# Throwaway products on TensorE in a fused mLSTM, routed-expert and soft-expert kernel, and late weight loads in column halves

## Chip, cores and metric

One Trainium2 chip, one core. The metric is device time in microseconds of one execution, as the median of several runs.

## The reference

Three stages, all in float32. Stage one is a gated linear-attention recurrence over 768 tokens, for 4 batches and 8 heads of 40 channels; stage two sends each of the 3072 tokens to one of 8 experts; stage three is a soft mixture over 32 slots.

```python
for t in range(S):                                    # stage one
    m_new = np.maximum(f_gate[:, :, t] + m, i_gate[:, :, t])
    C = f_stab * C + i_stab * outer(v_t, k_t);  n = f_stab * n + i_stab * k_t
    y_t = sigmoid(o_t) * (C @ q_t) / np.maximum(np.abs(n @ q_t), 1.0)
# stage two, x is (3072, 320)
expert_idx = np.argmax(x @ w_gate, axis=1)
out[mask] = gate_w[mask, None] * (np.maximum(x[mask] @ w1[e], 0.0) @ w2[e])
# stage three
logits = x @ phi                                      # (3072, 32)
slot_input = softmax(logits, axis=0).T @ x            # (32, 320)
slot_out[e] = np.maximum(slot_input[e] @ v1[e], 0.0) @ v2[e]   # 4 slots per expert
y = softmax(logits, axis=1) @ slot_out
```

w1 and v1 are 8 matrices of 320 x 1024, w2 and v2 of 1024 x 320.

## The kernel before

Each engine has its own hand-written program; semaphores join them. SyncE issues nearly all DMAs.

**Stage one** goes in 24 steps (6 chunks of 128 tokens by 4 batches, chunks outside). VectorE first works the gates through scans, from which it builds the operands of the first exponent product. For a step TensorE runs `exponents` (L1164, two products of 512 columns, whose results ScalarE puts through Exp and GpSimd masks), `scores` (L1176), `outputs` (L1187 for the carried state, from the second chunk on, and L1192), `new_state` (L1203) and `x_transpose` (L1209). VectorE weighs the scores with the decays (L883) before the outputs can run. After the first scores `gate_columns` transposes gate rows (L1245, L1248). Once in four steps come `router` (L1229) and `logit_transpose` (L1237).

**Routing** follows on one path through TensorE and VectorE: one-hot choice (`r_hot`), the rank products L1281 and L1282 (`r_rank`), positions and row masks on VectorE (L982), 24 slot products L1288 (`r_slots`), slot numbers to GpSimd, which gathers the rows of the tokens by indirect DMA; beside that the gate products L1374 (`slot_gates`, 10 of them before the first tile, 14 after its first layer).

**The expert loop** takes 31 tiles of 128 slots. Weights and activations are split in a high and a low fp32r part, and each product is made of three (L1315 to L1319 for layer 1, L1332 to L1334 for layer 2). It is the same before and after.

**The tail** is stage three: the column maximum (L1428, L1430), the slot inputs (L1437 over 31 tiles, four column tiles side by side, with the sums L1441 in between), a fold (L1447), then for two groups q of four experts `soft1` (L1461), `soft_transpose` (L1471), `soft2` (L1482), with `transpose_combine` (L1489) between the groups, a spreading product (L1502) and 24 final products L1511, which VectorE and ScalarE scale and SyncE stores.

The soft experts' weights go to places that become free: experts 6 and 7 into the places of experts 0 and 1, once `soft1(0)` has read them (`soft_h` at 2). `soft1(q)` waits for the whole w1 of its four experts and then makes the columns in two halves g of 512, each into a bank of its own. Before a stage's wait the program does nothing: `pe.wait_ge` stands there and TensorE is idle. Bank 6 is free until the first carried state, and again between the routing's products and the gates; bank 4 holds the ranks and, later, layer 2; bank 2 is free between the slot sums and the transposes.

The semaphore `consts` is raised by GpSimd as soon as the identity, the ones and `half` are made (L461 to L468).

Of the kernel before, what the change touches and what calls it, by code (L numbers as in the profile page):

```python
# [29 lines left out]
P = 128  # L30
# [16 lines left out]
def build(nc, i_gate, f_gate, qk_rows, kvo_rows, w_gate, phi, w1_main, w1_rest, w2, v1_main, v1_rest, v2, out):  # L47
    B, H, S = i_gate.shape
    DM, E = w_gate.shape
# [22 lines left out]
    with ExitStack() as ctx:  # L72
# [216 lines left out]
        soft_in = [[sem(f"soft_w1_in{n}"), sem(f"soft_w2a_in{n}"), sem(f"soft_w2b_in{n}")] for n in range(E)]  # L289
# [62 lines left out]
        def _(sp):  # L352
# [39 lines left out]
            def load_soft_w1(e):  # L392

                raw, there = soft_place(e), soft_in[e][0]
                sp.dma_start(raw[:, 0:2 * F], v1_main[e]).then_inc(there, 16)
                sp.dma_start(raw[0:KD[2][1], 2 * F:W1N], v1_rest[e]).then_inc(there, 16)

            def load_soft_w2(e, halves=(0, 1)):
                for x in halves:
                    a, z = x * W2N // 2, (x + 1) * W2N // 2  # L400
                    sp.dma_start(soft_place(e)[:, W1N + a:W1N + z], v2[e][:, a:z]).then_inc(soft_in[e][1 + x], 16)
# [40 lines left out]
            load_soft_w1(6)  # L442
            load_soft_w1(7)
# [705 lines left out]
        def _(pe):  # L1149
            mm = nc.tensor.matmul  # L1150
            tr = nc.tensor.transpose
            def exponents(i):

                c, b = ORDER[i]
                if c == 0:
                    pe.wait_ge(exp_first, 1)
                    pe.wait_ge(exp_const, 2)
                else:
                    pe.wait_ge(exp_next, c)
                    pe.wait_ge(exp_const, 4)  # L1160
                if i > 0:
                    pe.wait_ge(dec_raw, i)
                for a in range(2):
                    last = mm(bank[a][:, :], exp_cols[c % 2][:, b, :],  # L1164
                              exp_rows[c % 2][:, a * NP:(a + 1) * NP, :].rearrange("p n t -> p (n t)"), start=True, stop=True)
                last.then_inc(e_done, 1)
# [85 lines left out]
            pe.wait_ge(consts, 1)  # L1252
            exponents(0)
# [24 lines left out]

            pe.wait_ge(r_hot, 1)
# [3 lines left out]

            pe.wait_ge(r_row, 1)
# [93 lines left out]

            pe.wait_ge(r_gates_split, 1)
# [3 lines left out]
            gathered(0, 0, 0)  # L1383
            layer1(0, 0, at0)
# [41 lines left out]

            pe.wait_ge(cmax_in, 1)
            tr(bank[0][0:SLOTS, 0:P], cmx[:, :], ident[:, :]).then_inc(cmax_tr, 1)  # L1428
            pe.wait_ge(cmax_dg, 1)
            mm(bank[1][:, 0:SLOTS], ones[0:SLOTS, :], cdg[:, :], start=True, stop=True).then_inc(cmax_bc, 1)  # L1430
            pe.wait_ge(e_exp, 1)
            pe.wait_ge(y_kept, TILES)
            for j in range(TILES):
                if j == E_PARTS[1][0]:
                    pe.wait_ge(e_exp, 2)
                i = j % GRP * SLOTS
                last = mm(bank[3][i:i + SLOTS, 0:DM], et[:, j, :], ys3[:, j, :], start=(j < GRP), stop=(j >= TILES - GRP))  # L1437
                if j == TILES // 2:
                    pe.wait_ge(e_sum, 1)
                    for i in range(GRP):  # L1440
                        summed = mm(bank[2][i * SLOTS:(i + 1) * SLOTS, 0:1], esum[:, :], ones[:, 0:1], start=True, stop=True)  # L1441
                    summed.then_inc(sl_sum, 1)
# [8 lines left out]
            def soft1(q):  # L1451
                for e in range(GRP * q, GRP * (q + 1)):
                    pe.wait_ge(soft_in[e][0], 32)
                for g in range(2):
                    if q > 0:
                        pe.wait_ge(soft_relu[g], q)
                    for kk in range(3):
                        n = KD[kk][1]
                        for i in range(GRP):
                            e = GRP * q + i  # L1460
                            last = mm(bank[g][i * SLOTS:i * SLOTS + PER, :], s_T[0:n, kk, PER * e:PER * (e + 1)],  # L1461
                                      soft_place(e)[0:n, kk * F + g * 512:kk * F + (g + 1) * 512], start=(kk == 0), stop=(kk == 2))
# [11 lines left out]
            def soft2(q):  # L1474
                pe.wait_ge(hs_ready, 2 * q + 2)
                for kk in range(NF):
                    if kk % (NF // 2) == 0:
                        for e in range(GRP * q, GRP * (q + 1)):
                            pe.wait_ge(soft_in[e][1 + kk // (NF // 2)], 16)
# [15 lines left out]
            transpose_combine()  # L1495
            soft1(1)
# [48 lines left out]

# [26 lines left out]
```

## Time and profile before

| | us |
|---|---|
| median of 3 runs | 611.08 |
| lowest and highest run | 603.78, 613.95 |
| the profiled execution's own time | 603.99 |
| its span in the profile | 602.2 |
| TensorE busy | 523.0 (87%) |
| VectorE, ScalarE, GpSimd busy | 325.1, 194.1, 328.0 |
| mean granted TensorE clock | 0.921 |

The stages lie in the span thus: gates until 19.4, chunk steps until 203, routing until 228.6, expert loop until 537, tail until the end. A granted clock of 1.00 is 2.4 GHz, one of 0.50 is 1.2 GHz. The clock column has no level of its own for the time before the first recorded change, at 63.1 us, and shows 1.00 there; the lengths of the products tell it. An fp32 product appears as two records of TensorE; `x16` counts records.

### The profile page before, as it was taken

How to read it: one execution, taken by the hardware profiler on the slowest of the kernel's cores; microseconds unless marked ns; L12 is line 12 of the kernel's file. 1: busy time of each engine (PE TensorE's matmuls, PEld its weight loads, DVE VectorE, ACT ScalarE, POOL GpSimd, SP SyncE). 2: the span in 40 equal slices, each digit the busy share in tenths (PEclk: the TensorE clock that was granted, in tenths of full speed). 3: DMA queues.
4: the chain of work that ended last, by engine and by line, in shares of the span. 5: the costliest groups of instructions: out<-in, count | busy, mean ns of one | idle time of the engine just before them, and what ended most of it. 6: DMA issues, size and time to landing. Idle time of an engine off the chain costs nothing.

```text
span 602.2 us, 11312 instructions
## 1 busy us (share of the span) xinstructions
PE 523.0 (87%) x3819; PEld 443.8 (74%) x3820; DVE 325.1 (54%) x547; ACT 194.1 (32%) x424; POOL 328.0 (54%) x301
## 2 busy tenths in 40 slices
PE   0599999989999258999999999999999999979483
PEld 0389888878898146989898898989888989862222
DVE  7445677876744573634747757574554333342113
ACT  2233554646630221232333323232323232220003
POOL 2465768778644315755997868685297442102000
PEclk9999999999755557999999999999999999998887
DMA  6026789888720004348160606050230650039927
GB/s 207 0 67 218 222 264 272 266 260 266 232 86 22 11 18 114 89 111 223 68 213 16 208 22 202 22 202 22 90 117 20 213 182 16 2 114 359 340 92 262
DMA packets 28447, 86.22 MB, mean 143 GB/s; under 512 B 4464, under 2 KB 14816, under 8 KB 25344
## 3 DMA queue, kind: packets, MB, share of 16 engines
q1 hardware_dynamic: 21616, 75.07, 38.5%
q0 software_dynamic: 2480, 5.59, 3.7%
q10 hardware_dynamic: 4320, 5.15, 2.5%
q8 instruction: 20, 0.33, 0.2%
q14 instruction: 11, 0.09, 0.0%
HBM read 72.67 MB, written 8.37 MB: 135 GB/s over the span
## 4 chain that ended last, share of the span: by engine, by line
PE 73%; DVE 13%; issue 5%; DMA 4%; POOL 2%; ACT 1%; SPq 0%; DVEq 0%; ACTq 0%; POOLq 0%
PE bank L1192 8%; PE bank L1332 7%; PE bank L1334 6%; PE bank L1333 6%; PE bank L1315 5%; PE bank L1209 5%; PE bank L1317 4%; PE bank L1316 4%; PE bank L1176 4%; PE bank L1343 4%; PE bank L1187 3%; PE bank L1357 3%; DVE gates L1040 2%; PE bank L1319 2%; PE bank L1461 2%
## 5 line engine op out<-in xcount | busy, mean ns | idle before, releaser
L1332 PE MATMUL bank<-W_high,h_high 128*128 x248 | 79.1, 319 | 1.7 <-DVE h_low L1065 1.6
L626 POOL TENSOR_TENSOR W_high<-W,ones 128x3072 fp32r<-128x3072 f32 (+1 forms) x12 | 58.6, 4885 | 37.8 <-PE bank L1334 37.7
L1334 PE MATMUL bank<-W_low,h_high 128*128 x248 | 76.4, 308 | 0.0
L1333 PE MATMUL bank<-W_high,h_low 128*128 x248 | 76.4, 308 | 0.0
L592 POOL TENSOR_TENSOR W_low<-W,W_high 128x3072 fp32r<-128x3072 f32 (+1 forms) x12 | 74.9, 6238 | 0.9
L776 ACT ACTIVATE h_high<-bank 128x512 fp32r<-128x512 f32 x62 | 33.7, 595 | 123.7 <-PE bank L1343 119.5
L874 DVE RECIPROCAL hb<-hb 128x320 f32<-128x320 f32 x24 | 51.7, 2153 | 27.9 <-POOL hb L530 27.9
L635 POOL DMA_INDIRECT combine_slots<-gates,back_i x31 | 29.8, 960 | 60.3 <-ACT gates L764 37.3
L1192 PE MATMUL bank<-ys 128*128 128x41 f32 x384 | 59.4, 325 | 0.0
L1192 PEld LDWEIGHTS bank<-ys 128*128 128x128 f32 x384 | 57.9, 238 | 0.9 <-issue 0.9
L1315 PE MATMUL bank<-W_high,x_high 128*128 x124 | 52.8, 426 | 4.9 <-DVE x_high L1048 2.5
L1021 DVE TENSOR_TENSOR yc<-bank,slot_gate 128x320 f32<-128x320 f32 x31 | 15.2, 492 | 75.4 <-PE bank L1334 75.4
L1053 DVE TENSOR_SCALAR hb<-bank 128x512 f32<-128x512 f32 x31 | 21.3, 688 | 55.4 <-PE bank L1319 55.4
L1040 DVE TENSOR_TENSOR gates<-gates,rmx (+1 forms) x31 | 50.5, 1631 | 0.0
L1317 PE MATMUL bank<-W_low,x_high 128*128 x124 | 49.3, 398 | 0.0
L1316 PE MATMUL bank<-W_high,x_low 128*128 x124 | 49.3, 397 | 0.0
L1332 PEld LDWEIGHTS bank<-W_high,h_high 128*128 128x128 f32 x248 | 46.6, 188 | 2.4 <-issue 2.4
L1333 PEld LDWEIGHTS bank<-W_high,h_low 128*128 128x128 f32 x248 | 46.6, 188 | 0.0
L1334 PEld LDWEIGHTS bank<-W_low,h_high 128*128 128x128 f32 x248 | 46.5, 188 | 0.0
L609 POOL DMA_INDIRECT ys<-x_tokens,slot_i x29 | 32.2, 1112 | 25.7 <-DMA ys<-x_tokens,slot_i 22.8
L1065 DVE TENSOR_TENSOR h_low<-bank,h_high 128x512 fp32r<-128x512 f32 x62 | 39.7, 681 | 5.5 <-ACT h_high L776 5.5
L1176 PEld LDWEIGHTS bank<-ys 48*128 48x128 f32 x384 | 30.5, 238 | 13.7 <-issue 11.4
(245 smaller groups left out, 1090.6 us busy)
## 6 DMA issues: line engine op xcount, KB each, us to landing
W<-in_moe_w_main_dram SPq DMA_DIRECT2D x13, 1024.0 KB, 6.0
ys<-in_kvo_rows_dram SPq DMA_DIRECT2D x24, 484.0 KB, 5.5
ys<-in_qk_columns_dram SPq DMA_DIRECT2D x24, 448.0 KB, 4.2
W<-in_moe_w_rows_dram SPq DMA_DIRECT2D x8, 1280.0 KB, 9.2
W<-in_moe_w_rows_dram SPq DMA_DIRECT2D x10, 640.0 KB, 8.8
W<-in_moe_w_rest_dram SPq DMA_DIRECT2D x21, 256.0 KB, 6.7
xs<-ys ACTq DMA_DIRECT2D x29, 160.0 KB, 2.1
x_tokens<-xs SPq DMA_DIRECT2D x24, 160.0 KB, 4.9
```

Source lines behind the costliest of these rows:

```text
L592: g.tensor_tensor(W_low[:, w], W[:, w], W_high[:, columns(e % 2, part_)].bitcast(F32), ALU.subtract).then_inc(w_split[part_], 1)
L626: g.tensor_tensor(W_high[:, columns(e % 2, part_)], w, ones[:, 0:1].broadcast_to(list(w.shape)), ALU.mult).then_inc(high_ready, 1)
L874: v_.reciprocal(eo[i % 3], eo[i % 3]).then_inc(recip_ready, 1)
L1040: v_.tensor_tensor(a(cexp), a(lg2), m.unsqueeze(2).broadcast_to([P, 1, SLOTS]), ALU.subtract).then_inc(c_in, 1)
L1176: last = mm(bank[3 + a][:, n * P:(n + 1) * P], qkT[i % 3][r, 1, n, :], qkT[i % 3][r, 0, n, :], start=True, stop=True)
L1192: last = mm(bank[5][:, h * DA:(h + 1) * DA], pr[i % 2][h % 2][:, h // 2, :], vt[i % 3][:, h, :], start=True, stop=True)
L1315: mm(dst, x_high[n][:, kk, :], high, start=(kk == 0), stop=False)
L1316: mm(dst, x_low[n][:, kk, :], high, start=False, stop=False)
L1317: mm(dst, x_high[n][:, kk, :], w1_at(W_low, slot, kk, half_, P), start=False, stop=False)
L1332: mm(dst, h_high[:, kk, :], high, start=(kk == 0), stop=False)
L1333: mm(dst, h_low[:, kk, :], high, start=False, stop=False)
L1334: last = mm(dst, h_high[:, kk, :], w2_at(W_low, slot, kk), start=False, stop=(kk == NF - 1))
```

## The change

A helper is added to TensorE's program. It multiplies the identity by the identity, repeated four times to 512 columns, into a bank whose content nobody reads:

```diff
+            def keep_warm(n, free):
+                for _ in range(n):
+                    mm(free[:, :], ident[:, :], ident[:, :].unsqueeze(1).broadcast_to([P, 4, P]), start=True, stop=True)
...
             pe.wait_ge(consts, 1)
+            keep_warm(28, bank[6])
             exponents(0)
...
+            keep_warm(5, bank[6])
             pe.wait_ge(r_hot, 1)
...
+            keep_warm(14, bank[6])
             pe.wait_ge(r_row, 1)
...
+            keep_warm(8, bank[6])
             pe.wait_ge(r_gates_split, 1)
             slot_gates(0, 10)
             fetch(0)
             at0 = places(expert[0])
             gathered(0, 0, 0)
+            keep_warm(3, bank[4])
             layer1(0, 0, at0)
...
+            keep_warm(1, bank[2])
             pe.wait_ge(cmax_in, 1)
...
+            keep_warm(1, bank[2])
             pe.wait_ge(e_exp, 1)
...
                 if j == E_PARTS[1][0]:
+                    keep_warm(2, bank[2])
                     pe.wait_ge(e_exp, 2)
...
             transpose_combine()
+            keep_warm(10, bank[2])
             soft1(1)
```

These are 72 products. Where they stand on TensorE, at the start of its program (`bank<-ident` is the throwaway; L1164 before is L1170 now), before:

```order
L1148 UNCONDITIONAL_BRANCH
L1164 MATMUL bank<-exp_rows_53,exp_cols_55 128x512 x4
L1176 MATMUL bank<-ys 128x128 x8
L1245 MATMUL bank<-ident,gates 128x32 x12
L1248 MATMUL bank<-gates,half 128x96 x2
```

and now:

```order
L1149 UNCONDITIONAL_BRANCH
L1156 MATMUL bank<-ident 128x512 x28
L1170 MATMUL bank<-exp_rows_53,exp_cols_55 128x512 x4
L1182 MATMUL bank<-ys 128x128 x8
L1251 MATMUL bank<-ident,gates 128x32 x12
L1254 MATMUL bank<-gates,half 128x96 x2
```

All 28 stand ahead of the first exponent products; nothing else moved. The routing on TensorE, from the last logit transpose to the first layer-1 product, before:

```order
L1237 MATMUL bank<-ident,sin_ 128x128
L1281 MATMUL bank<-oh_bf,before_bf 128x192
L1282 MATMUL bank<-oh_bf,ones_bf 128x192
L1288 MATMUL bank<-token_hot,rowhot 128x64 x24
L1374 MATMUL bank<-gate_parts,rowhot 128x64 x10
L1365 TENSOR_LOAD eot_i
L1209 MATMUL bank<-ident,xs 128x128 x3
```

and now:

```order
L1243 MATMUL bank<-ident,sin_ 128x128
L1156 MATMUL bank<-ident 128x512 x5
L1289 MATMUL bank<-oh_bf,before_bf 128x192
L1290 MATMUL bank<-oh_bf,ones_bf 128x192
L1156 MATMUL bank<-ident 128x512 x14
L1297 MATMUL bank<-token_hot,rowhot 128x64 x24
L1156 MATMUL bank<-ident 128x512 x8
L1383 MATMUL bank<-gate_parts,rowhot 128x64 x10
L1374 TENSOR_LOAD eot_i
L1215 MATMUL bank<-ident,xs 128x128 x3
L1156 MATMUL bank<-ident 128x512 x3
```

Four groups of throwaways stand in the four waits. The other part of the change is the soft experts' w1. On the host its main part is laid out so that the first 512 columns of both row blocks come before the last 512. Each w1 is loaded by four DMAs instead of two, halves apart, and for experts 6 and 7 the first halves of both go first. For experts 4 to 7 each half has a semaphore of its own, and `soft1` waits for a half before the product g that reads it:

```diff
-            def load_soft_w1(e):
-
-                raw, there = soft_place(e), soft_in[e][0]
-                sp.dma_start(raw[:, 0:2 * F], v1_main[e]).then_inc(there, 16)
-                sp.dma_start(raw[0:KD[2][1], 2 * F:W1N], v1_rest[e]).then_inc(there, 16)
+            def load_soft_w1(e, halves=(0, 1)):
+                for x in halves:
+                    a, there = x * W1N // 2, soft_in[e][2 + x * (e // GRP)]
+                    sp.dma_start(soft_place(e)[:, a:a + F], v1_main[e][:, x * F:(x + 1) * F]).then_inc(there, 16)
+                    sp.dma_start(soft_place(e)[0:KD[2][1], a + F:a + W1N // 2], v1_rest[e][:, x * F // 2:(x + 1) * F // 2]).then_inc(there, 16)
...
             sp.wait_ge(soft_h, 2)
-            load_soft_w1(6)
-            load_soft_w1(7)
+            for x in range(2):
+                load_soft_w1(6, (x,))
+                load_soft_w1(7, (x,))
...
             def soft1(q):
-                for e in range(GRP * q, GRP * (q + 1)):
-                    pe.wait_ge(soft_in[e][0], 32)
                 for g in range(2):
+                    for e in range(GRP * q, GRP * (q + 1)):
+                        pe.wait_ge(soft_in[e][2 + q * g], 32 if q else 64)
```

## Rows read from the trace of the kernel before

**Rows 1.** Windows cut where the granted clock changes: busy us of each engine, PEclk, DMA share, GB/s

```profile
29.60:63.10 33.50, 33.47 (x218) 29.37 (x220) 17.77 (x24) 12.98 (x29) 20.49 (x41) 1.00 0.45 143
63.10:158.70 95.60, 88.87 (x1047) 78.73 (x1047) 71.74 (x107) 51.01 (x118) 72.00 (x113) 1.00 0.85 263
158.70:203.30 44.60, 38.81 (x236) 33.58 (x235) 20.44 (x27) 11.82 (x25) 24.33 (x27) 0.50 0.20 66
203.30:233.80 30.50, 14.28 (x51) 12.17 (x52) 18.75 (x49) 8.29 (x8) 7.51 (x7) 0.50 0.14 38
...
541.00:547.80 6.80, 5.78 (x54) 2.37 (x56) 2.24 (x4) 1.21 (x3) 4.35 (x8) 0.50 1.01 368
...
568.30:575.10 6.80, 3.60 (x20) 0.52 (x24) 0.00 (x0) 0.00 (x0) 0.00 (x0) 0.50 1.00 363
```

**Rows 2.** Timeline of GpSimd, first 3 us: start, length, what

```profile
2.46 0.14 POOL L468 MEMSET half<- 32x64 f32 x1
```

**Rows 3.** Timeline of TensorE, 18 to 62 us

```profile
19.36 1.19 PE L1164 MATMUL bank<-exp_rows,exp_cols 128*128 128x512 f32 x2 [19.36 <-DVE exp_cols L859]
...
29.63 2.08 PE L1176 MATMUL bank<-ys 48*128 48x128 f32 x16 [1.08 <-DVE ys L883]
31.64 3.63 PE L1192 MATMUL bank<-ys 128*128 128x41 f32 x16
```

**Rows 4.** The chain that ended last: start, length, what

```profile
20.59 1.09 ACT arena L656 x2
...
28.20 1.30 DVE ys L883 x2
...
64.55 1.75 PE bank L1192 x16
...
67.84 1.09 PE bank L1176 x16
...
161.39 2.01 PE bank L1176 x16
...
170.20 2.01 PE bank L1176 x16
```

**Rows 5.** Timeline of TensorE, chunk boundaries, 80 to 160 us

```profile
106.76 0.30 PE L1237 MATMUL bank<-ident,sin_ 128*128 128x128 f32 x1 [1.05 <-issue]
...
155.73 0.30 PE L1237 MATMUL bank<-ident,sin_ 128*128 128x128 f32 x1 [1.04 <-issue]
```

**Rows 6.** Timeline of TensorE, products of the tail, 551 to 587 us

```profile
551.38 0.60 PE L1461 MATMUL bank<-W,s_T 128*4 128x512 f32 x2 [0.41 <-DVE s_T L1123]
...
551.82 0.59 PE L1461 MATMUL bank<-arena,s_T 128*4 128x512 f32 x1
...
585.86 0.81 PE L1502 MATMUL bank<-gates,spread 128*128 128x320 f32 x2 [0.62 <-DVE gates L1139]
```

**Rows 7.** Timeline of TensorE, the routing

```profile
206.59 0.34 PE L1281 MATMUL bank<-oh_bf,before_bf 128*128 128x192 bf16 x1 [3.38 <-DVE oh_bf L948]
...
214.83 5.30 PE L1288 MATMUL bank<-token_hot,rowhot 128*128 128x64 f32 x24 [7.75 <-DVE rowhot L982]
222.52 2.34 PE L1374 MATMUL bank<-gate_parts,rowhot 128*128 128x64 f32 x10 [2.39 <-DVE gate_parts L1007]
225.99 0.90 PE L1209 MATMUL bank<-ident,xs 128*128 128x128 f32 x3 [1.12 <-DMA xs<-x_tokens,slot_i]
228.57 0.79 PE L1315 MATMUL bank<-W_high,x_high 128*128 x1 [1.68 <-DVE x_high L1048]
```

**Rows 8.** Timeline of TensorE, start of the tail

```profile
538.23 0.28 PE L1428 MATMUL bank<-ident,cmx 128*32 128x128 f32 x1 [0.51 <-DVE cmx L1097]
...
540.34 0.73 PE L1437 MATMUL bank<-ys,gates 128*32 128x320 f32 x4 [0.83 <-ACT gates L798]
542.09 3.95 PE L1437 MATMUL bank<-ys,gates 128*32 128x320 f32 x26 [1.02 <-ACT gates L798]
```

**Rows 9.** Timeline of TensorE, second w1 product of the tail

```profile
571.50 1.01 PE L1461 MATMUL bank<-arena,s_T 128*4 128x512 f32 x1 [7.27 <-DMA W<-in_moe_w_rest_dram]
```

More of the change, by code:

```diff
@@ L288, in build @@
         weights_in = sem("weights_in")
-        soft_in = [[sem(f"soft_w1_in{n}"), sem(f"soft_w2a_in{n}"), sem(f"soft_w2b_in{n}")] for n in range(E)]
+        soft_in = [[sem(f"soft_{part_}_in{n}") for part_ in ("w2a", "w2b", "w1a", "w1b")[:3 + n // 4]] for n in range(E)]
         dve_chain = sem("dve_chain")
@@ L400, in load_soft_w2 @@
                     a, z = x * W2N // 2, (x + 1) * W2N // 2
-                    sp.dma_start(soft_place(e)[:, W1N + a:W1N + z], v2[e][:, a:z]).then_inc(soft_in[e][1 + x], 16)
+                    sp.dma_start(soft_place(e)[:, W1N + a:W1N + z], v2[e][:, a:z]).then_inc(soft_in[e][x], 16)
             def load_soft(e):
@@ L1461, in soft1 @@
                             last = mm(bank[g][i * SLOTS:i * SLOTS + PER, :], s_T[0:n, kk, PER * e:PER * (e + 1)],
-                                      soft_place(e)[0:n, kk * F + g * 512:kk * F + (g + 1) * 512], start=(kk == 0), stop=(kk == 2))
+                                      soft_place(e)[0:n, g * W1N // 2 + kk * 512:g * W1N // 2 + (kk + 1) * 512], start=(kk == 0), stop=(kk == 2))
                     last.then_inc(soft_h, 1)
@@ L1478, in soft2 @@
                         for e in range(GRP * q, GRP * (q + 1)):
-                            pe.wait_ge(soft_in[e][1 + kk // (NF // 2)], 16)
+                            pe.wait_ge(soft_in[e][kk // (NF // 2)], 16)
                     for i in range(GRP):
@@ L1543, in _token_rows, with _by_column_halves @@
     return np.ascontiguousarray(np.concatenate([a.reshape(a.shape[0], P, -1) for a in parts], axis=2))
+def _by_column_halves(rows, parts):
+    split = rows.reshape(rows.shape[0], rows.shape[1], parts, 2, -1).transpose(0, 1, 3, 2, 4)
+    return np.ascontiguousarray(split.reshape(rows.shape))
 def kernel(**inputs):
@@ L1560 @@
         a = _np.asarray(inputs[first])
-        laid.append((first + "_main", _partition_rows(a[:, :2 * P])))
+        main = _partition_rows(a[:, :2 * P])
+        laid.append((first + "_main", _by_column_halves(main, 2) if first == "moe2_w1" else main))
         laid.append((first + "_rest", _np.ascontiguousarray(a[:, 2 * P:])))
```

## The prediction

> **What bounds the kernel now.** I read the page's 40 slices first, then a table of windows cut where the granted clock changes, then TensorE's timeline at each place where the change adds work. TensorE is 87% busy and the chain that ended last runs over it, so its speed decides. That speed is not constant. The windows [rows 1] show the clock at 1.00 from 63.1 to 158.7 us, 0.50 until 233.8, 1.00 through the expert loop, and two short stretches of 0.50 in the tail. Before 63.1 the column says 1.00 too, but there the records contradict it: the same sixteen products of L1192 take 3.63 us at 31.6 and 1.75 us at 64.6 [rows 3, 4]. So TensorE runs at 1.2 GHz until 63.1 and at 2.4 GHz after it. A chunk step takes 8.8 us at the lower level (two starts of L1176, 161.4 and 170.2) and at the higher 49.0 us for the eight steps between the logit transposes at 106.76 and 155.73, 6.1 each [rows 4, 5]. In the low stretch 29.6 to 63.1 TensorE is busy 33.47 of 33.50 us [rows 1]: there it is the bound, and a faster clock pays at once.
>
> **The sum's base.** The profiled execution took 603.99 us (span 602.2, 1.8 around it). The median shown is 611.08, 7.1 more, and the three runs lie 10.2 apart. Four steps at 8.8 instead of 6.1 are 10.8 us, so one chunk more or less at the low clock explains the spread. 2% of the median, about what a measurement of this kernel can tell from no change, is 12.2 us: faster means below 598.9, slower above 623.3.
>
> **What one throwaway costs.** No row shows it. The nearest is the one untiled fp32 product of 320 columns, L1502: two records that take 0.82 us together [rows 6]; the shorter of them lasts 0.43, so they start 0.39 apart, which is 0.62 for 512 columns if none of it is start-up. In L1461, with 512 columns and four small tiles side by side, the next pass over the same tile starts 0.44 us after the first (551.38 and 551.82) [rows 6]. I take 0.43 us per record and two records per product: 0.85 us at 2.4 GHz, 1.7 us at 1.2. The bounds are 0.43 (if one record did) and 1.24 (two records 0.62 apart). The identity is fp32, as L1502's operands are, so 0.85 is nearest.
>
> **Front, 28 of them.** They start when the fourth small memset is done at 2.6 us [rows 2] and stand ahead of exponents(0), which now starts at 19.36, released by VectorE. The first stretch of dense work after a low clock shows when it rises: from 228.57 to 233.8 is 5.2 us, from 571.5 to 575.1 is 3.6 us [rows 1, 7, 9]. I take 4.5 us, 2.6 products; the other 25.4 take 21.7 us. TensorE is free at 28.9 us, that is +9.5 us. (At 2.4 GHz throughout 26.6; at 1.24 each about 37.) Behind it the startup runs faster. Now 19.36 to 29.63 is 10.3 us: product, ScalarE's exponential, product, scores, gate columns, two copies and a weighing on VectorE [rows 3, 4]. With TensorE's pieces halved it is 0.6 + 1.1 + 0.6 + 1.1 + 1.2 + 0.2 + 0.8 + 1.3 = 6.9, so -3.4. Then five steps lie between the scores of step 1 at 29.63 and those of step 6 at 67.84: 38.2 us [rows 3, 4]. At the high clock a step costs at least 3.8 (half of 38.2 / 5) and at most the 6.1 of a later chunk, which has L1187 besides. I take 5.2: 26.0 us, -12.2. Front: 9.5 - 3.4 - 12.2 = -6.1 us, bounds -14 and 0.
>
> The cover of this term is the clock itself. From 4.8 us after the 28 until 6.9 us after them TensorE waits for VectorE, an idle of 2.1 us where it was 1.08, because the wait is VectorE's and does not shrink. The clock has gone through idles of 1.05 us at 105.7 unharmed and fell at 158.7 after one of 1.04 [rows 5]. The Trainium skill ("TensorE: Matmul & The Clock Gate", Part 4) says that transposes do not count as busy for the clock. Were that so here, the 12 gate-column transposes would lengthen the gap from the scores on, and the front would end at +6.2 instead of -6.1; no row separates transposes from the rest.
>
> **Chunk loop.** No instruction changes. I leave the fall at the end of the fifth chunk where it is: 0, with 0 to -14 if it does not fall (rival C).
>
> **Routing, 5 + 14 + 8 + 3.** TensorE's waits here are 3.38, 7.75, 2.39 + 1.12 and 1.68 us [rows 7]. The 5 start at 203.2 at the low clock: 4.5 us for 2.6 of them and 2.4 x 0.85 for the rest, 6.5 us, done at 209.7 against 206.6: +3.1, and the rank product and all of VectorE's chain behind it (7.95 us to the first rowhot) are late by that. The 14 take 11.9 us from 210.0, done at 221.9, while VectorE has its quarter ready at 217.9. The 24 slot products take 5.30 us now; at the high clock 2.7: 224.6 against 220.1, +4.5. The 8 take 6.8, the ten gate products 1.2: 232.6. The gathered rows come 5.9 us after the slots (220.1 to 226.0), at 230.5, so they are hidden. Three transposes 0.5 and the 3 throwaways 2.6: layer 1 starts at 235.7, +7.1 against 228.57. Its first ten or so products now take 5.2 us until the clock rises and will take 2.6. Net +4.5 us (bounds: -3 if everything fits in the waits, +7 if the clock is low again). The expert loop follows at 1.00 either way: shifted, not changed.
>
> **Tail, 1 + 1 + 2 + 10 and the halves.** The waits are 0.51, 0.83 and 1.02 us [rows 8]; against 0.85, 0.85 and 1.7 this delays by 0.3 + 0 + 0.7. In return the clock stays up where it is 0.50 from 541.0 to 547.8 [rows 1], and the L1437 groups (8 groups of four tiles, about 7.3 us with the sums between) take some 4.7: -2.6. Net about -1.6 before soft1(0). soft1(1) now waits 7.27 us, until 571.5, for the last rest load of w1 [rows 9]. The 10 take 8.5 us from 562.6, until 571.1; the first column halves of experts 6 and 7 have come by then, since the queues are full (1.02 of 16 engines) and half of the 2.5 MB is left. The second halves are there at about 571.3, as the whole was, and are wanted only 2.6 us later. soft1(1) takes 5.2 instead of 7.4 us and ends at 576.2 instead of 579.0: -2.8 us for the whole tail (the 1.6 is inside it). Bounds 0, if smaller packets slow the loads, and -5, if g = 0 could start early. SyncE issues 16 DMAs more, some 0.5 us each, while its queues hold work: nothing. What ends the kernel stays the output's transfer.
>
> **Sum.** 603.99 - 6.1 + 0 + 4.5 - 2.8 = 599.6 us for an execution whose chunk loop goes as the profiled one did. The median of before sits 7.1 higher for a rise that came late or a fall that came early; the 28 remove the first kind only. I add a third, 2.4: forecast 602.0, own range 593 to 609.
>
> **Rivals.**
> B, the clock falls in the startup gap. For: 2.1 us idle, twice today's, with little work ahead of it; the fall at 158.7 needed only 1.04 us and a thin stretch of L1192 behind it. Against: the same idle at 105.7 did nothing. The 28 then bought nothing: scores 1 at 35.8 instead of 29.63, +6.2, and the cold steps as now: 602 + 12.3 = 614. If the rise that came at 63 then comes a chunk later, 10.8 more: 625. It decides from the first fall before 40 us on. This is the one that ends slower than before.
> C, the clock does not fall at 158.7, since the phase of every idle has moved. Four steps at 6.1 instead of 8.8 and a quicker router, some 12.5 us, and the 5 throwaways enter at the high clock, 2.2 less: 602 - 15 = 587. For it: the boundary idles of the other chunks passed. Against it: nothing in the change touches this stretch.
> D, the throwaways are short, so they don't do what they say. At the lower bound, one record each, the 28 end near 13 to 15 us, the idle until 19.36 is over 4 us, and the clock fell in the idle after 564.2 after 4.1 us [rows 1, 9]. Nothing is gained in front, the routing's fit in the waits and cost nothing; tail -2.8, layer 1 -1.3: 611.1 - 4.1 = 607. The skill's same page (section on the back-to-back issue gap) gives N/2.4 + 2.5 ns, 0.216 us for 512 columns, which would put the 28 at under 10 us and the result at the same 607; the records of L1502 speak against it, and another page, "FP8 and Floating Point Precision", counts four passes for true fp32.
>
> **Chances.** Forecast 0.37; B 0.30, of it 0.11 beyond 623; C 0.18; D 0.07; the rest, mixtures such as a fall at the first chunk boundary (near 606 to 616), 0.08. Faster by over 2%: C, and a third of the forecast's own range, 0.30. Slower by over 2%: 0.12. Within: 0.58. The range leaves out the far ends of B and C: 587 to 621.
>
> **What would show it.** Right: L1164's first start near 29, L1192 at 1.75 us per sixteen from its first step on, scores 6 near 61, rank product 3 us behind the router, layer 1 some 7 us after today's distance from the router, soft1(1) done at the high clock. Wrong: throwaways that end the 28 before 20 us (D); L1192 at 3.6 us per sixteen in the first steps (B); windows at 1.00 up to the router (C). If the routing's waits still stand in the list of waits, my throwaway is too long by half.

## The result, and the profile after

| | before | after |
|---|---|---|
| median, us | 609.41 | 629.38 |
| lowest and highest of 4 runs, us | 603.78, 613.95 | 626.24, 639.45 |
| after / before | | 1.034, 95% interval 1.022 to 1.046 |

The change makes the kernel slower, by 20 us between the medians. The forecast was 602.0 us within 587 to 621. The profiled execution of after is the longest of its four, 639.45 us; the other three took 626 to 631. So its stages are read one by one below, and its chunk loop is not typical. The ratios with an interval, here and below, are taken from the fast runs alone, so they are not the quotients of the medians beside them, which are of all runs.

The page of after first. TensorE is busy for 76.8 us more than before, 68.5 of them the throwaways' own (144 records, 72 products), and the chain that ended last runs over those for 9% of the span.

```profile
span 637.6 us, 11620 instructions
...
PE 599.8 (94%) x3963; PEld 485.7 (76%) x3964; DVE 331.7 (52%) x547; ACT 195.1 (31%) x424; POOL 327.7 (51%) x301
...
PEclk9965569855559869999999999999999999999998
...
PE 82%; DVE 7%; issue 4%; DMA 2%; POOL 2%; ACT 1%; SPq 1%; DVEq 0%; POOLq 0%; ACTq 0%
...
L1156 PE MATMUL bank<-ident 128*128 128x512 f32 x144 | 68.5, 631 | 3.7 <-POOLq L470 2.7
```

Then the windows of after, cut where the granted clock changes, which answer to [rows 1] (columns: window, length, then busy us and number of records of TensorE, its weight loads, VectorE, ScalarE, GpSimd; clock; DMA share; GB/s). The column to look at is the clock: it rises at 8.0, while the 28 throwaways run, falls at 35.3, six microseconds after them, and stands at 0.50 until 89.9. Before, the low stretch ended at 63.1. It is low again from 124.0 to 192.3, with TensorE busy for 68.30 of 68.30 us. From 265.4 on it stays up until 632.6, through nearly the whole tail, where before it fell three times.

```profile
8.00:35.30 27.30, 25.91 (x89) 12.53 (x87) 12.09 (x15) 6.04 (x10) 8.06 (x16) 1.00 0.20 48
35.30:89.90 54.60, 53.16 (x338) 47.00 (x340) 28.01 (x40) 19.08 (x42) 32.83 (x59) 0.50 0.44 137
89.90:124.00 34.10, 32.14 (x387) 28.50 (x384) 25.09 (x38) 17.11 (x42) 23.81 (x38) 1.00 0.83 271
124.00:192.30 68.30, 68.30 (x457) 60.18 (x456) 34.40 (x50) 24.37 (x54) 34.87 (x55) 0.50 0.51 161
192.30:232.50 40.20, 32.23 (x321) 27.93 (x322) 24.66 (x34) 16.29 (x34) 26.82 (x32) 0.88 0.38 129
232.50:265.40 32.90, 31.88 (x100) 16.24 (x100) 18.74 (x49) 7.75 (x7) 6.56 (x6) 0.94 0.09 24
265.40:575.00 309.60, 302.69 (x1875) 271.69 (x1874) 168.75 (x283) 93.96 (x214) 188.91 (x78) 1.00 0.33 105
575.00:632.60 57.60, 48.17 (x402) 19.39 (x400) 14.94 (x34) 9.18 (x22) 4.36 (x8) 1.00 0.83 271
```

By stages, each from its first product to that of the next, in us of the profiled executions:

| stage | before | after | difference | forecast |
|---|---|---|---|---|
| start to scores of step 1 | 29.6 | 36.7 | +7.1 | +6.1 |
| scores of step 1 to last logit transpose | 173.1 | 195.5 | +22.4 | -12.2 |
| last logit transpose to layer 1 (routing) | 25.8 | 33.2 | +7.3 | +7.1 |
| layer 1 to column maximum (expert loop) | 309.7 | 309.7 | 0.0 | -2.6 |
| column maximum to end (tail) | 64.0 | 62.6 | -1.4 | -2.8 |
| span | 602.2 | 637.6 | +35.4 | |

(The routing's three parts are, before and after, 3.9 and 6.7 to the rank product, 8.2 and 11.8 to the slot products, 13.7 and 14.7 to layer 1. The table's rows add up to the span within rounding.)

### The profile page after: what moved, and what is told of

Its sections match the earlier page's. It is cut to its first block, busy times and chain, and to the rows that moved or that the text cites. A ratio compares the mean times of both kernels' runs of the same rounds, so it can differ in the third digit from the quotient of the medians.

```text
span 637.6 us, 11620 instructions
## 1 busy us (share of the span) xinstructions
PE 599.8 (94%) x3963; PEld 485.7 (76%) x3964; DVE 331.7 (52%) x547; ACT 195.1 (31%) x424; POOL 327.7 (51%) x301
## 4 chain that ended last, share of the span: by engine, by line
PE 82%; DVE 7%; issue 4%; DMA 2%; POOL 2%; ACT 1%; SPq 1%; DVEq 0%; POOLq 0%; ACTq 0%
PE bank L1156 9%; PE bank L1198 8%; PE bank L1341 6%; PE bank L1343 6%; PE bank L1342 6%; PE bank L1182 5%; PE bank L1324 5%; PE bank L1215 5%; PE bank L1326 4%; PE bank L1325 4%; PE bank L1193 4%; PE bank L1352 3%; PE bank L1366 3%; DMA W<-in_moe_w_rest_dram 2%; DVE gates L1041 2%
## 5 line engine op out<-in xcount | busy, mean ns | idle before, releaser
L1156 PE MATMUL bank<-ident 128*128 128x512 f32 x144 | 68.5, 631 | 3.7 <-POOLq L470 2.7
L1198 PE MATMUL bank<-ys 128*128 128x41 f32 x384 | 66.1, 347 | 0.0
L1198 PEld LDWEIGHTS bank<-ys 128*128 128x128 f32 x384 | 64.8, 263 | 0.9 <-issue 0.9
L1156 PEld LDWEIGHTS bank<-ident 128*128 128x128 f32 x144 | 28.5, 203 | 37.2 <-issue 34.8
L1041 DVE TENSOR_TENSOR gates<-gates,rmx (+1 forms) x31 | 56.6, 1830 | 0.0
L1182 PEld LDWEIGHTS bank<-ys 48*128 48x128 f32 x384 | 35.1, 270 | 15.2 <-issue 14.5
```

The lines of the kernel that those rows point to most:

```text
L1041: v_.tensor_tensor(a(cexp), a(lg2), m.unsqueeze(2).broadcast_to([P, 1, SLOTS]), ALU.subtract).then_inc(c_in, 1)
L1156: mm(free[:, :], ident[:, :], ident[:, :].unsqueeze(1).broadcast_to([P, 4, P]), start=True, stop=True)
L1182: last = mm(bank[3 + a][:, n * P:(n + 1) * P], qkT[i % 3][r, 1, n, :], qkT[i % 3][r, 0, n, :], start=True, stop=True)
L1198: last = mm(bank[5][:, h * DA:(h + 1) * DA], pr[i % 2][h % 2][:, h // 2, :], vt[i % 3][:, h, :], start=True, stop=True)
```

## The experiments

Sixteen kernels. Each is the kernel before with the helper and the edits named (e9 is the kernel after, e5 has no helper); e1 to e4 also mask the expert number that TensorE's loop reads (`pe.snap(e & 7)`), e5 to e16 instead hold the tile-to-expert table as 16-bit numbers. Neither changes a product or a load. e5 is the second edit alone, the control; the mask has no control of its own. Kernels of one group ran on one chip, with the kernel before beside them. The text of each expectation is as it was written before the run.

### One part at a time

e1 has the front's 28 alone, e2 the routing's four calls alone, e3 the tail's four and the column halves (as in the change's diff, whose other lines for the tail are left out):

```diff
# e1
             pe.wait_ge(consts, 1)
+            keep_warm(28, bank[6])
             exponents(0)
# e2
+            keep_warm(5, bank[6])
             pe.wait_ge(r_hot, 1)
...
+            keep_warm(14, bank[6])
             pe.wait_ge(r_row, 1)
...
+            keep_warm(8, bank[6])
             pe.wait_ge(r_gates_split, 1)
...
+            keep_warm(3, bank[4])
             layer1(0, 0, at0)
# e3
             transpose_combine()
+            keep_warm(10, bank[2])
             soft1(1)
```

> Only the 28 throwaways ahead of the first exponent product; the rest is the kernel before (as in all kernels of this study, the expert number that two waits compare against is masked with 7, one register operation more). Theory A (the clock falls in the startup gap and the chunk loop then runs longer at 1.2 GHz): first L1164 near 29 us, granted clock 0.50 by 40 us, rise not before 60 us, +10 to +20 us against before. Theory B (only the overrun counts, the clock in the loop is what it was): +6 to +7 us. The forecast on record would want -6.

> Only the 5 + 14 + 8 + 3 throwaways of the routing. Overrun as in the forecast: layer 1 starts about 7 us later after the router than before, +4 to +7 us in all. If they fitted in the waits: 0 to -3 us. Theory A gives nothing more here, as the chunk loop is over.

> Only the tail: 1 + 1 + 2 + 10 throwaways and the loads in halves. The forecast's term: -2.8 us, clock at 1.00 from the first tail product to the output. If the 10 overrun what they win: 0 to +2 us.

The fourth, e4, tests the cover that the prediction named for its front term: 16 throwaways, which fit the wait, and three more that fill the two waits behind them.

```diff
+            keep_warm(16, bank[6])
             exponents(0)
...
+                if i == 0:
+                    keep_warm(1, bank[5])
                 if i + 1 < NT:
                     exponents(i + 1)
+                if i == 1:
+                    keep_warm(2, bank[5])
                 if i < NT:
                     scores(i)
```

> 16 throwaways in front instead of 28 (2.6 + 4.5 + 13.4 x 0.85 = 18.5 us, under the 19.4 us of the wait), and 1 behind the first exponent pair and 2 ahead of the scores of step 1, where TensorE waits 1.3 and 2 us. Theory A: the clock holds through the startup, scores of step 1 near 26.5 us, scores of step 6 near 53, -5 to -14 us against before, less what later falls take. Theory B (the loop's clock has nothing to do with the gap): scores of step 1 the same 26.5, but the clock at 0.50 within some 10 us of it; -2 to 0 us.

| | median, us | range, runs |
|---|---|---|
| before | 622.92 | 601.09 to 642.82, 7 |
| e1 | 630.77 | 615.73 to 652.74, 4 |
| e2 | 631.32 | 624.83 to 643.24, 4 |
| e3 | 616.77 | 614.87 to 630.24, 5 |
| e4 | 621.52 | 619.64 to 627.42, 4 |

The medians are of little use: the kernel before itself spreads over 42 us here. The traces say more. e1 has scores 1 at 36.1 and the clock fall at 33.96, as in after, but the clock is up again at 61.3, where after has 89.9. e2 has the routing's stages of after (6.4, 11.8, 14.7 us). e3 takes 63.2 us from the column maximum to the end; after takes 62.6.

e4 is the one that decides. TensorE's timeline of e4, to be held against [rows 3]:

```profile
2.70 16.53 PE L1155 MATMUL bank<-ident 128*128 128x512 f32 x32 [2.70 <-POOLq L469]
...
25.03 1.88 PE L1155 MATMUL bank<-ident 128*128 128x512 f32 x4
26.84 1.16 PE L1181 MATMUL bank<-ys 48*128 48x128 f32 x16
...
31.09 1.16 PE L1181 MATMUL bank<-ys 48*128 48x128 f32 x16
...
34.93 1.06 PE L1169 MATMUL bank<-exp_rows,exp_cols 128*128 128x512 f32 x2 [0.17 <-POOL exp_cols L539]
35.92 2.08 PE L1181 MATMUL bank<-ys 48*128 48x128 f32 x16
37.93 3.63 PE L1197 MATMUL bank<-ys 128*128 128x41 f32 x16
```

The waits are full now but for 0.41 us, scores 1 stands at 26.84, and scores 2 and 3 follow 4.3 and 4.8 us apart instead of 7.74, at the high clock. Then the clock falls all the same, at 35.14: L1181 takes 1.16 us at 31.09 and 2.08 at 35.92. By its windows TensorE was busy for 8.13 of the 8.30 us from 26.84 on. So a filled startup does not keep the clock up. It falls in the chunk steps themselves, which are busy nearly throughout by the records but made of short pieces: the longest line of a step, L1197, is sixteen records of 41 columns, each behind a weight load of its own. That the short pieces are the reason is an assumption; no run varies them alone, and in before the steps after 63.1 us, made of the same lines and L1187 besides, kept the clock up for 95.6 us.

### Fillers in the steps

e5 is the control. e6 has e4's edits and a filler in every step: `half_warm`, one product of 256 columns, in `new_state` after its waits, and in `x_transpose` in the steps that make no new state; and one throwaway at each chunk boundary. e7 has the routing with 3, 8, 4 and 1, e8 the tail with 1, 1, 1 and 7 and the column halves.

```diff
# e6
+            def half_warm(free):
+                mm(free[:, 0:2 * P], ident[:, :], ident[:, :].unsqueeze(1).broadcast_to([P, 2, P]), start=True, stop=True)
...
                     pe.wait_ge(state_ready, i)
+                half_warm(bank[7])
...
+                if i + 3 > STATES:
+                    half_warm(bank[2])
...
                 if i >= 8 and (i - 3) % B == 1:
+                    pe.wait_ge(o_read, i - 1)
+                    keep_warm(1, bank[6])
                     logit_transpose((i - 3) // B - 1)
# e7, ahead of the wait for r_row
+            keep_warm(8, bank[6])
# e8
             transpose_combine()
+            keep_warm(7, bank[2])
             soft1(1)
```

> The kernel before with one edit that all kernels of this study need: the expert number that TensorE loads for its waits is stored as a 16-bit unsigned number here, where the first four kernels masked it with 7. The first four showed a wait of 5 to 10 us of TensorE inside the expert loop some 75 us before its end. If the mask's extra register operation made it, it is gone here and the kernel takes the time of before (ratio 1.00); if it stays, it is the chip's.

> 16 throwaways in front, 1 and 2 in the two startup waits, 1 in the wait at each chunk boundary, and one of 256 columns (0.43 us) in each of the 24 steps, in front of the state products or of the last transposes. Theory A (thin stretches of L1192 and L1203 let the clock fall in the loop): clock at 1.00 from 8 us to the last logit transpose or nearly, that transpose near 175 to 185 us instead of 202.7, total 15 to 25 us below before. Theory C (the clock toggles for other reasons): low stretches of 40 us and more remain in the loop, and the 24 x 0.43 = 10 us are lost: +5 to +10 us.

> 3 + 8 + 4 + 1 throwaways in the routing, sized by the measured 0.854 us of one and a rise after some 4 us. If the overrun was the whole cost of the routing's 30: the way from the last logit transpose to layer 1 takes 25.9 us before, 33.1 with 5 + 14 + 8 + 3, and 23 to 27 here; 0 to -3 us in all.

> Tail with 1 + 1 + 1 + 7 throwaways and the loads in halves. If the 10 held soft1(1) back (they ended when it began): it starts 19 us after soft1(0) instead of 21.4, when the first halves are there, and the tail from the column maximum to the end takes 60 to 61 us against 64.0 before; if the loads decide, 21 us and 62 to 63.

| | median, us | range, runs |
|---|---|---|
| before | 626.97 | 607.72 to 648.60, 7 |
| e5 | 618.79 | 611.09 to 634.46, 4 |
| e6 | 601.75 | 592.47 to 612.67, 4 |
| e7 | 628.93 | 609.97 to 651.59, 6 |
| e8 | 620.80 | 611.26 to 644.63, 4 |

In e6, whose front is that of e4, the clock is at 1.00 from 6.8 to 177.5 us without a break, and the stretch from scores 1 to the last logit transpose takes 155.4 us, where the six traces without throwaways in front or fillers (before, e2, e3, e5, e7, e8) have 171.6 to 185.9, 176.5 in the mean. At the high clock the filler makes a step 0.5 us longer (scores 1 to scores 2 take 4.76 us in e6 and 4.25 in e4), but the loop is 21 us shorter.

e7 fits the counts to the waits: the slots are at 4.7 + 8.1 us instead of 6.4 + 11.8, but layer 1 comes 16.0 us after them instead of 14.7, so the routing takes 28.7 us: still more than the 25.8 of before. TensorE's timeline of e7 shows where:

```profile
228.44 3.37 PE L1295 MATMUL bank<-token_hot,rowhot 128*128 128x64 f32 x24 [0.86 <-DVE rowhot L982]
235.16 6.13 PE L1155 MATMUL bank<-ident 128*128 128x512 f32 x8 [3.35 <-DVEq L1005]
```

Behind the slot products the program waits for `routed`, which VectorE raises at L1005, and only then come the throwaways that were meant for the wait for the gates. TensorE idles 3.35 us there, the clock falls at 233.3, and the four throwaways hold up the gate products until 240.73, 5.6 us where four at the high clock take 3.4. The eight of the change stand in the same place.

e8 has the 7 throwaways end just as the first halves of the second group's w1 land:

```profile
583.05 6.17 PE L1156 MATMUL bank<-ident 128*128 128x512 f32 x14
589.66 0.59 PE L1470 MATMUL bank<-arena,s_T 128*4 128x512 f32 x1 [0.43 <-DMA W<-in_moe_w_rest_dram]
```

TensorE waits 0.43 us there, where it waited 7.27 before [rows 9] and not at all in after, and 1.74 us more between its two halves, for the second halves of the load. From the column maximum to the end e8 takes 62.1 us.

### After again, and the fillers with the tail or without the front

e9 is the whole changed kernel. e10 is e6 with the tail of e8. e11 is e6 without the 16 and the three in front, so fillers and chunk boundaries alone. e12 is e6 with fillers of 128 columns:

```diff
# e11, against e6
-            keep_warm(16, bank[6])
             exponents(0)
# e12, against e6
-                mm(free[:, 0:2 * P], ident[:, :], ident[:, :].unsqueeze(1).broadcast_to([P, 2, P]), start=True, stop=True)
+                mm(free[:, 0:P], ident[:, :], ident[:, :], start=True, stop=True)
```

> The changed kernel whole, with the 16-bit expert number, beside the kernel before on the same chip. Front 28 leave scores of step 1 at 36.7 us against 29.6, the routing from the last logit transpose to layer 1 takes 33 us against 26: +13 us are laid down by overruns less 1 in the tail. Theory A adds 5 to 15 us for the loop's low clock after a fall near 35 us: 1.02 to 1.04 of before. If the overruns are all: 1.02.

> e6 (fillers in every step, 16 in front, startup waits and boundaries) together with e8 (tail 1 + 1 + 1 + 7, halves). Theory A: the clock holds in the loop again, last logit transpose at 176 to 186 us; column maximum to end 60 to 62 us against 64; 20 to 28 us below before. Theory C (e6 was luck): loop as before, +5.

> Only the fillers in the steps and at the boundaries, none in front. Theory A: TensorE starts at 1.2 GHz, and with 0.85 us more dense work in a step at that clock the rise comes earlier than 55 to 63 us and then holds: last logit transpose near 190 us, 10 to 18 us below before. If the front is what counts and not the steps: no gain, 0 to +8.

> e6 with fillers of 128 columns (some 0.21 us) instead of 256 in the steps. If this still holds the clock, the loop is 24 x 0.21 = 5 us shorter than in e6; if not, low stretches of 30 us and more are back in the loop and it takes 5 to 20 us longer than e6.

| | median, us | range, runs | ratio to before, 95% |
|---|---|---|---|
| before | 611.21 | 598.06 to 632.09, 13 | |
| e9 | 620.36 | 613.52 to 636.71, 4 | 1.034 (1.009 to 1.059) |
| e10 | 586.70 | 580.43 to 591.71, 4 | 0.970 (0.957 to 0.983) |
| e11 | 602.71 | 595.95 to 608.98, 10 | 1.002 (0.995 to 1.008) |
| e12 | 583.76 | 581.45 to 585.51, 4 | 0.973 (0.965 to 0.981) |

e9 is slower than before again, by a ratio near that of the first measurement, but the medians of all its runs and of before's lie only 9.2 us (1.5%) apart. Its chunk loop is another: 170.7 us where after has 195.5, and yet the first fall and the rise behind it are the same (35.67 and 90.28). Its span is 611.7, 26 us less, and 25 of them are the loop's luck.

e12 holds the clock with half the filler. TensorE's timeline of a step of e12, in which the filler is L1158, 0.47 us by its two records. It moves the next product by 0.29 us: L1200 and L1212 start 2.14 apart, where the same lines of after are 1.85 apart at the high clock (98.01 and 99.86):

```profile
103.51 1.92 PE L1200 MATMUL bank<-ys 128*128 128x41 f32 x16
105.25 0.47 PE L1158 MATMUL bank<-ident 128*128 128x128 f32 x2
105.65 0.67 PE L1212 MATMUL bank<-ys 128*64 128x41 f32 x16
```

And its windows:

```profile
8.40:42.55 34.15, 32.36 (x233) 21.09 (x233) 23.25 (x32) 13.36 (x26) 22.40 (x46) 1.00 0.42 124
42.55:52.80 10.25, 10.25 (x71) 8.99 (x69) 7.03 (x10) 5.96 (x14) 7.86 (x15) 0.50 0.64 186
52.80:172.30 119.50, 117.29 (x1296) 101.71 (x1294) 89.83 (x133) 61.16 (x138) 90.90 (x134) 1.00 0.73 231
```

One low stretch of 10.3 us is left before the last steps; from 172.3 to 209.8, in the last steps and the routing, the clock is low again. The first stretch follows a wait of 1.38 us for VectorE at 42.3, but e15 (below), which has the same steps and a wait of 1.37 us in the same place, kept the clock up until 165. e11 shows that the fillers alone aren't enough: its first rise comes at 65.35, as before's does, and only then do they hold the clock (until 195). Nor is the warm front alone (e4). Both together are, for most of the loop. How much of that is due to the products at the chunk boundaries or in the two startup waits no run tells.

### The counts around the fillers

e13 is e12 again, e15 is e12 with the four calls of e2 in the routing, e16 is e12 with the tail of e8 (1, 1, 1, 7 and the column halves), and e14 has 28 in front:

```diff
# e14, against e12
-            keep_warm(16, bank[6])
+            keep_warm(28, bank[6])
             exponents(0)
```

> The kernel of e12 again, as the base of the three beside it on the same chip: its loop holds the clock, its runs lay within 4 us of each other, so that overruns can be read without the loop's chance. 580 to 590 us if the chip makes no stall in the expert loop, up to 10 more if it does.

> e13 with 28 in front instead of 16, so that TensorE comes to the first exponents near 29 us instead of 19.4 to 20. Overrun theory: +9 to +10.5 us against e13 (12 x 0.854 = 10.2). Forecast on record, where the front's delay is won back by the high clock: in e13 the clock is high already, so this asks for the price of the delay alone. If the others' work in the meantime pays some of it back: +5 or less.

> e13 with the routing's 5 + 14 + 8 + 3. Overrun theory: last logit transpose to layer 1 33 us instead of 26, +6 to +7.5 us against e13, less nothing in the expert loop. If layer 1 and its expert loop win it back at the high clock: 0 to +3.

> e13 with the tail's 1 + 1 + 1 + 7 and the loads in halves. -1 to -3 us against e13, by the time from the column maximum to the end (63 us without, 62 and less with); 0.96 to 0.98 of before.

| | median, us | range, runs | ratio to before, 95% |
|---|---|---|---|
| before | 613.12 | 597.82 to 637.84, 7 | |
| e13 | 584.36 | 577.93 to 591.23, 4 | 0.974 (0.956 to 0.992) |
| e14 | 591.58 | 589.55 to 595.01, 4 | 0.984 (0.971 to 0.997) |
| e15 | 587.08 | 583.21 to 590.79, 4 | 0.973 (0.955 to 0.991) |
| e16 | 583.23 | 579.18 to 589.61, 4 | 0.966 (0.954 to 0.979) |

With the clock held the scatter is smaller, but e13 still ranges over 13 us. The 28 cost 7.2 us against the 16 by the medians (e14 and e13), and in the traces scores 1 stands at 36.9 and 26.9, which is ten of the 12.6 us by which their spans differ. The routing's thirty throwaways cost 7.3 us in the trace of e15 (33.3 against 26.0 us), of which the medians show 2.7, within their scatter. The tail of e8 brings nothing that the medians can tell (e16 and e13: -1.1), and its length in the traces scatters as that of the others does: 62.1 in e8, 67.0 in e10, 63.6 in e16. Nor do the fillers hold the clock in every execution alike: early in the loop it was low for 10.3 us in e12, 6.8 in e13, 10.2 in e14, 27.3 in e16 and not at all in e15. e12, e13 and e16 are faster than before, and e12 than the whole change on its chip (e9) as well; between the three nothing is settled.

## Why the prediction was wrong

**The step that failed: the five steps behind scores 1, "I take 5.2: 26.0 us, -12.2".** The 28 were to buy a startup and five steps at the high clock. TensorE's timeline of after, beside [rows 3]:

```profile
2.71 26.91 PE L1156 MATMUL bank<-ident 128*128 128x512 f32 x56 [2.71 <-POOLq L470]
29.06 1.03 PE L1170 MATMUL bank<-exp_rows,exp_cols 128*128 128x512 f32 x2
31.36 0.70 PE L1170 MATMUL bank<-exp_rows,exp_cols 128*128 128x512 f32 x2 [1.27 <-ACT arena L657]
...
36.74 2.08 PE L1182 MATMUL bank<-ys 48*128 48x128 f32 x16 [1.56 <-DVE ys L884]
38.74 3.63 PE L1198 MATMUL bank<-ys 128*128 128x41 f32 x16
...
44.47 2.08 PE L1182 MATMUL bank<-ys 48*128 48x128 f32 x16
```

The 28 end at 29.6 and L1170 starts at 29.06 (forecast 28.9), the clock is up from 8.01, and the pieces behind them are shorter: L1170 takes 0.70 us at 31.36 where it took 1.19. The wait for VectorE ahead of scores 1 is 1.56 us, shorter than the 2.1 that the working expected. So the startup came nearly as forecast: the delay is 9.7 us (forecast 9.5), the startup behind it takes 7.7 instead of 10.3, a return of 2.6 (forecast 3.4), and scores 1 stands 7.1 late (forecast 6.1). But at 35.3 the clock falls, scores 1 at 36.74 takes 2.08 again and scores 2 comes 7.73 us later, at 44.47, the same low-clock step as before. The five steps from scores 1 to scores 6 take 42.0 us in after and in e9 and 34.4 in e1, where the six kernels with neither front nor fillers have 34.3 to 42.0. They returned nothing that can be told from the kernel's own spread, where 12.2 us were forecast.

The size of the term was not the fault: in e15, where the clock stays up from 8.0 to 165 us, the same five steps take 27.1 us with a filler in each (forecast 26.0 without). What failed is that the clock would stay up through them. Rival B had the place and the price right (+6.2, scores 1 at 35.8, the fall before 40 us). The idle that it gave as the cause is not needed: in e4, with the waits full, the clock fell all the same, at 35.14, two steps past scores 1. What the prediction lacked is that [rows 1] showed TensorE 33.47 of 33.50 us busy at the low clock, before any rise. These steps, busy throughout, ran for 33 us without raising the clock, and the working took for granted that they would keep it up.

The Trainium skill ("TensorE: Matmul & The Clock Gate", Part 4) gave another cause for the same end, that transposes do not count for the clock. In e4 the clock passed the gate-column transposes at 23.1 to 24.0 and fell eleven microseconds later, with only products and weight loads in between. The rule isn't needed for what the traces show, and no run here tests it.

**Low-clock steps were priced too low.** I took 8.8 us, from two steps late in the kernel, where `new_state` (L1203) is no longer run. In the chain of after the same line starts 10.1 and 10.0 us apart:

```profile
158.72 2.01 PE bank L1182 x16
...
168.81 2.01 PE bank L1182 x16
...
176.09 1.01 PE bank L1209 x16
...
178.79 2.01 PE bank L1182 x16
```

L1209 (L1203 before) is 1.01 us of it. Such a step at the low clock costs 10.0 us, and four of them over a chunk boundary 41.5 in after, against four times 6.1 at the high clock. So a later chunk more or less is 17 us, not 10.8. A few of them are the kernel's own spread: the 34 executions of before beside the experiments range from 597.8 to 648.6 us, and their time mostly falls as their mean granted clock rises (correlation -0.72; 601 us at 0.937, 643 and 644 at 0.860 and 0.871, but one of 638 at 0.941).

**Chunk loop, forecast 0.** In after's profiled execution it cost +22.4. Of the three traces with the 28 but no fillers the stretch is 162.7 (e1), 170.7 (e9) and 195.5 us (after), 176.3 in the mean; of the six without, 171.6 to 185.9 and 176.5. So nothing systematic is seen, though three traces that spread over 33 us would not show a few microseconds: the rise and fall of the clock in the loop differ between executions, and after's was a bad draw. Rival C had the fall at 158.7 for its subject; in after the clock falls at 124.1, 212.8 and 226.5 instead.

**Throwaway, 0.85 us: right.** Fourteen of them hold TensorE from 239.05 to 250.70 (fence of the routing, below), 0.83 each; the ten of the tail from 599.07 to 607.75, 0.87 each. Rival D is out. The Trainium skill ("FP8 and Floating Point Precision", TensorE Precision Notes) counts four passes for true fp32; four times 512 columns at 2.4 GHz make an estimate of 0.853 us, and the trace agrees.

**Routing, forecast +4.5: right in the delays, wrong in what comes back.** TensorE's timeline of after, beside [rows 7]:

```profile
232.24 0.47 PE L1243 MATMUL bank<-ident,sin_ 128*128 128x128 f32 x1 [0.40 <-ACT sin_ L694]
232.51 6.54 PE L1156 MATMUL bank<-ident 128*128 128x512 f32 x10
238.89 0.25 PE L1289 MATMUL bank<-oh_bf,before_bf 128*128 128x192 bf16 x1
...
239.05 12.21 PE L1156 MATMUL bank<-ident 128*128 128x512 f32 x28
250.70 3.16 PE L1297 MATMUL bank<-token_hot,rowhot 128*128 128x64 f32 x24
254.88 7.11 PE L1156 MATMUL bank<-ident 128*128 128x512 f32 x16 [1.02 <-DVEq L1006]
261.42 1.60 PE L1383 MATMUL bank<-gate_parts,rowhot 128*128 128x64 f32 x10
...
263.24 2.74 PE L1156 MATMUL bank<-ident 128*128 128x512 f32 x6
265.42 0.79 PE L1324 MATMUL bank<-W_high,x_high 128*128 x1
```

and VectorE's, the operands of the gate products:

```profile
254.84 0.96 DVE L1008 TENSOR_TENSOR gate_parts<-ys,gate_parts 128x768 fp32r<-128x768 f32 x1 [0.16 <-DVE slot_i L1005]
```

The five take until 238.9, and the rank product is 6.65 us after the logit transpose instead of 3.86: +2.8 (forecast +3.1). The fourteen run 12.21 us by their records where VectorE needed 8: the slots are another 3.6 late, +6.4 (forecast +7.1). At the high clock the 24 slot products take 3.16 instead of 5.30, but the eight run until 261.42, and layer 1 starts +7.3 late (forecast +7.1). The waits of 7.75, 2.39 and 1.68 us are gone, but for 1.02, which is the wait for `routed` ahead of the eight: all were filled beyond their length. The eight were the worst placed. Of the 2.39 us of before only the last 1.0 was the wait for the gates that they stand ahead of (VectorE works these from 221.51 to 222.47); in after the gates are ready at 255.8, and the eight hold TensorE until 261.42. The return of 2.6 us in the first products is there at first, the second layer 1 comes 7.83 us after the first instead of 9.91, 2.1 sooner. Over the whole expert loop nothing is left of it in after and 1.0 us in e9 (308.7 against 309.7); where it is lost was not traced. So the term is +7, not +4.5.

**Tail, forecast -2.8: of the right sign, too large.** TensorE's timeline of after, beside [rows 8, 9]:

```profile
576.28 1.12 PE L1156 MATMUL bank<-ident 128*128 128x512 f32 x2
577.33 0.73 PE L1451 MATMUL bank<-ys,gates 128*32 128x320 f32 x4
577.99 1.98 PE L1156 MATMUL bank<-ident 128*128 128x512 f32 x4
579.91 2.08 PE L1451 MATMUL bank<-ys,gates 128*32 128x320 f32 x26
...
599.07 8.75 PE L1156 MATMUL bank<-ident 128*128 128x512 f32 x20
607.75 0.59 PE L1475 MATMUL bank<-arena,s_T 128*4 128x512 f32 x1
...
611.53 0.59 PE L1475 MATMUL bank<-arena,s_T 128*4 128x512 f32 x1 [0.92 <-DMA W<-in_moe_w_rest_dram]
```

The clock does stay up, and L1451's groups take 2.08 us instead of 3.95; soft1(0) comes 1.8 us sooner after the column maximum (11.3 against 13.1; forecast 1.6). The ten then take until 607.75, and soft1(1) starts after them without any wait, 21.4 us after soft1(0) where it was 20.1. With seven (e8) it is 19.3, and a DMA ends the wait.

What the working had wrong here is the load. It had the second halves land when the whole w1 did, 19.9 us after soft1(0) began. In after they land 24.9 us after it (the first halves at 20.4), and soft1(1) waits 0.92 us for them at 611.5, between its two halves. In the six traces with loads in halves the last weights land 23.7 to 27.1 us after soft1(0), in the twelve without 18.1 to 22.4. The last of the eight issues stands 2.3 us later than the last of the four did (9.6 against 7.3 us after soft1(0)); why the rest is lost is open, and the halves were not run without the throwaways. So soft1(1) ends 28.0 us after soft1(0) began where it was 27.5, and the early start is used up. From its start to the first final product 0.7 us come back (15.1 against 15.8). Net -1.4. But this stage takes 62.1 to 67.0 us, 64.6 in the mean, in the twelve traces whose tail is not changed, and 62.6, 63.2 and 63.4 in the three with the change, so -1.5 in the mean, and inside the spread.

**The sum.** Front +7, routing +7, tail -1.5, expert loop 0 to -1, loop 0: about +12, 2.0% of 609. Measured is +20, with an interval of 2.2% to 4.6%. e9 gives 0.9% to 5.9% by its ratio and 1.5% by the medians of all runs, which hold the +12. What lies between +12 and +20 can be the chunk loop's luck over eight executions or a loss that three traces don't show; that stays open. Right in the prediction were the base, the throwaway, the delays and most of the startup; wrong were the terms that were to pay for them, the five steps above all, then the routing's return and half of the tail's gain. The chance of 0.12 for slower by over 2% was too low, because rival B kept the routing's return and the tail's gain whole. With those at what they measured it is 602 + 12.3 + 2.8 + 1.3 = 618. Both traces of the whole change have the rise a chunk later (89.9 and 90.3, not 63.1), which costs after 8.3 us more against before by scores 8 (95.5 against 80.1, less the 7.1 of the start; rival B had 10.8): 627, near the measured 629. That fit is luck in part: e1, with the same front, has its rise at 61.3, and e7 and e8, without any front, at 83.1 and 84.9.

## What to carry to other kernels

A warm-up of the clock pays only if what follows keeps the clock up, and a high busy share in the records doesn't promise that: look at what the clock did in the same stage the last time TensorE was equally busy there. Here a product of 128 columns in every step, 0.3 us each, together with a warm-up no longer than the wait that it fills, made the kernel about 3% faster, while 72 long throwaways in the waits made it 3% slower (1.5% in the second measurement, by the medians of all runs). Count the throwaways from the wait's measured length and round down; each one too many moves the chain behind it by its own 0.85 us. Look in the program which wait they stand ahead of, and whether another one comes before them. And when a load is cut into pieces, read when the last piece lands, not only the first.

## What the hardware showed that was not expected

The clock fell with TensorE 98% busy ahead of the fall (e4, 8.13 of 8.30 us before 35.14), and stayed low in after with TensorE busy 68.30 of 68.30 us. With one product added to each step, 0.5 us of a step of some 6, and the startup filled, it stood at 1.00 for 170 us (e6). The kernel's time is thereby uncertain by itself: before varies by 51 us over those 34 executions on four chips, e12 by 4 and e13 by 13 over four executions each.

In the traces of e1 to e8 the expert loop takes 320 to 328 us instead of 309.7. Part of the excess, 5.4 to 9.8 us, is one pause of TensorE, which begins between 451 and 496 us. TensorE, VectorE and ScalarE stop and go on together. VectorE's timeline of e5, the control, shows it:

```profile
470.42 0.19 DVE L1029 TENSOR_TENSOR gates<-bank,pen 128x32 f32 x1 [1.82 <-remote]
...
479.07 0.49 DVE L1021 TENSOR_TENSOR yc<-bank,slot_gate 128x320 f32<-128x320 f32 x1 [8.15 <-remote]
```

The release is put down as remote, and GpSimd's descriptors go on through it. It is in none of e9 to e16, nor in before or after. e5 changes the width of a table alone and was no slower than before on its chip, and before itself had medians of 623 and 627 on those two chips against 609 to 613 on the others. So it seems to belong to the chip or the session rather than to an edit; no trace of before was taken there, and its cause stays open. No conclusion above rests on these expert loops.
